# All filters and seven weight chunks loaded behind the input, the turn done by quarter products, and GpSimd's weight work moved behind the units

## The chip, the cores and the metric

The program runs on one NeuronCore of a Trainium2 chip. The metric is the device time of one execution in microseconds (us), lower being better. Matrix products run on TensorE (PE, with its weight loads as PEld), copies and elementwise work on VectorE (DVE), ScalarE (ACT) and GpSimd (POOL), and the transfers are issued mostly by SyncE (SP).

## What is computed

```python
X = np.fft.rfft(x, axis=1)                      # x: 2 x 3008 x 256
F = (filt_r + 1j * filt_i)[None, :, :]
y = np.fft.irfft(X * F, n=3008, axis=1)         # then 6016 x 256
h = y @ w_in1;  g = np.maximum(0.01 * h, h);  z = g @ w_out1    # 256 -> 2048 -> 256
h = z @ w_in2;  r = np.maximum(h, 0.0);  out = (r * r) @ w_out2
```

A filter in the frequency domain over the sequence, and two feed-forward layers behind it, all in fp32.

## The kernel before, in words

**The filter stage.** The transform of length 3008 is made of one of length 64 (N1) and one of length 47 (N2). It has these steps:

- `over_n1`: 24 groups of four fp32 products of 128x128 over the input X, written to PSUM and copied to `TT1A` (by ACT) and `TT1B` (by DVE). These arrays have two halves in their partitions (0 to 63 and 64 to 127).
- sixteen units, each of which takes eight columns of `TT1` through four steps. `turn(i)` brings the sequence index into the partitions: eight transposes against the identity, `DM[:, 2, :]`, four for each batch b, into PSUM banks 0 and 1. ACT copies the banks to S2 (`turned(i)`, line 529). `spectrum(i)` (lines 954 to 957) is four fp32 products of 48 rows and 64 columns of weights over 512 columns, one in each quarter of the array. DVE multiplies by the filter (`filtered(i)`, lines 762 and 766), POOL combines (lines 449 and 450), `inverse(i)` (lines 974 to 977) is again four quarter products, and ACT copies the result to U (`back(i)`, line 537). SP stores U to DRAM (`zu`).
- `sequence(c)` (line 997): c from 0 to 23, four fp32 products of 128x128 each, over tiles V that are loaded from `zu`. Their results are copied to YT by DVE (`Y_DVE`) and ACT (`Y_ACT`). The second half (c from 12) needs the last unit's store and a load behind it.

The order in which PE runs the units is written out by hand: in each iteration i stand `spectrum(i + 2)`, `turn(i + 3)` and `inverse(i)`, from i = 13 on with some `sequence` calls in place of the turn. ACT's order beside it is `turned(i + 3)`, then `back(i)`.

**The layers.** The products run as three fp32r passes (high and low parts of each operand) by a fast scheme with seven forms of each block of weights and tokens. For the first layer POOL makes four sums for each weight chunk k (`wi_sums`, lines 357 to 363), ACT or DVE rounds the chunk (`wi_round`), and POOL takes the low parts (`wi_split`, line 369, three instructions). The forms of the first token pair are made by DVE (lines 807 to 818) and split by `x_split0` (lines 792 and 795); each of them has to be there before a certain step of PE: `x0_lo` counts them. A slot s is one weight chunk against one pair: `up_1(s)`, `up_2(s)`, `up_6(s)`, `up_7(s)`, `up_5(s)` and `group_d(s)` (lines 1029 to 1031), with `down` (lines 1021 to 1023) some steps behind. There are 96 slots of about 10 us.

**Loads.** SP's queue runs in order. Before, it issues the input, tables and the weight chunks 0 and 1, six filters into a ring of six (`FL`), and then one filter, the unit's stores and now and then a weight chunk for each unit.

**Beside the units.** POOL makes the sums and low parts of chunks 0, 1 and the sums of chunk 2 between the units, and everything of chunks 3 to 6 right behind the last unit.

## Time and profile before

| | us |
|---|---|
| median of three runs | 1069.74 (1068.79 to 1070.24) |
| the profiled execution, device time | 1068.72 |
| its span in the trace | 1066.7 |
| PE busy in the span | 1059.6 |
| DVE, ACT, POOL busy | 755.7, 564.7, 300.7 |

TensorE had its full clock (2.4 GHz) in all forty slices of the profile. The layers take from about 101 us to the end; all that the change touches on the critical chain lies before about 107 us. A busy share says which engine has work, and the chain of waits which one sets the end: by the page, PE is 98% of it.

### The profile page before, as it was taken

What the parts mean: (1) busy time and instruction counts of PE and PEld (TensorE: products, weight loads), DVE (VectorE), ACT (ScalarE), POOL (GpSimd) and SP (SyncE); (2) the same over time, 40 slices, a digit from 0 to 9 for tenths busy, and PEclk for the clock granted to TensorE, in tenths of its full rate; (3) what the DMA queues carried; (4) which work ended last, traced back from release to release, by engine and by line L of the source; (5) the groups of instructions that cost most, each with busy time, mean ns of one, the idle gap of its engine ahead of it and who ended that gap; (6) DMA issues with size and microseconds to landing.
All of it is one profiled execution on the core that took longest, in us unless ns stands there. A gap on an engine that the chain in (4) does not pass through costs nothing.

```text
span 1066.7 us, 13987 instructions
## 1 busy us (share of the span) xinstructions
PE 1059.6 (99%) x5120; PEld 880.0 (83%) x5120; DVE 755.7 (71%) x1141; ACT 564.7 (53%) x980; POOL 300.7 (28%) x287
## 2 busy tenths in 40 slices
PE   9998999999999999999999999999999999999998
PEld 9558888888888888888999888888888888888998
DVE  2877997767767777676666767667667676676666
ACT  3666554655555555554554544544554554554443
POOL 2997552342342333332220220220220210210000
PEclk9999999999999999999999999999999999999999
DMA  9696000112112112112244000100100100100100
GB/s 321 179 298 224 10 1 1 52 36 61 47 35 68 40 42 67 38 45 57 93 160 163 21 1 1 40 1 1 40 1 1 40 1 1 40 1 1 40 1 35
DMA packets 66724, 61.45 MB, mean 58 GB/s; under 512 B 40688, under 2 KB 53856, under 8 KB 66656
## 3 DMA queue, kind: packets, MB, share of 16 engines
q1 hardware_dynamic: 66160, 60.06, 18.1%
q8 instruction: 41, 0.67, 0.3%
q10 hardware_dynamic: 496, 0.49, 0.1%
q14 instruction: 27, 0.22, 0.1%
HBM read 36.55 MB, written 23.99 MB: 57 GB/s over the span
## 4 chain that ended last, share of the span: by engine, by line
PE 98%; DVE 1%; DMA 1%; ACT 0%; issue 0%; POOL 0%; SPq 0%; DVEq 0%; ACTq 0%; POOLq 0%
PE PS L1021 16%; PE PS L1023 16%; PE PS L1022 16%; PE PS L1029 14%; PE PS L1031 14%; PE PS L1030 14%; PE PS L913 2%; PE PS L937 2%; PE PS L977 1%; PE PS L957 1%; PE PS L997 1%; DMA V<-zu 0%; PE PS L903 0%; DMA zu<-U 0%; DVE YL L792 0%; DVE XL L795 0%
## 5 line engine op out<-in xcount | busy, mean ns | idle before, releaser
L666 ACT ACTIVATE GH<-GF 128x512 fp32r<-128x512 f32 (+1 forms) x384 | 238.7, 622 | 228.0 <-DVE GF L856 116.3
L862 DVE TENSOR_TENSOR GL<-GF,GH 128x512 fp32r<-128x512 f32 (+1 forms) x384 | 260.6, 685 | 105.2 <-ACT GH L666 99.5
L1021 PE MATMUL PS<-GH,WOH 128*128 128x512 f32 (+1 forms) x768 | 296.2, 386 | 0.0
L1022 PE MATMUL PS<-GL,WOH 128*128 128x512 f32 (+1 forms) x768 | 295.8, 385 | 0.0
L1023 PE MATMUL PS<-GH,WOL 128*128 128x512 f32 (+1 forms) x768 | 295.8, 385 | 0.0
L1029 PE MATMUL PS<-XH,WIH 128*128 128x512 f32 (+1 forms) x672 | 259.8, 387 | 2.3 <-DVE XL L795 1.4
L1031 PE MATMUL PS<-XH,WIL 128*128 128x512 f32 (+1 forms) x672 | 258.8, 385 | 0.0
L830 DVE TENSOR_TENSOR GF<-PS,GF 128x512 f32<-128x512 f32 (+1 forms) x96 | 65.3, 680 | 161.7 <-ACT GF L637 161.4
L1021 PEld LDWEIGHTS PS<-GH,WOH 128*128 128x128 f32 x768 | 144.2, 188 | 28.0 <-DVE GL L862 1.5
L1023 PEld LDWEIGHTS PS<-GH,WOL 128*128 128x128 f32 x768 | 144.2, 188 | 26.9
L1022 PEld LDWEIGHTS PS<-GL,WOH 128*128 128x128 f32 x768 | 144.2, 188 | 26.8
L1029 PEld LDWEIGHTS PS<-XH,WIH 128*128 128x128 f32 x672 | 126.2, 188 | 27.1 <-DVE XL L795 1.1
L1030 PE MATMUL PS<-YL,WIH 128*128 128x512 f32 (+1 forms) x384 | 147.8, 385 | 0.0
L1031 PEld LDWEIGHTS PS<-XH,WIL 128*128 128x128 f32 x672 | 126.2, 188 | 23.6
L854 DVE SCALAR_TENSOR_TENSOR GF<-GF 128x512 f32<-128x512 f32 (+1 forms) x192 | 144.0, 789 | 1.6
L637 ACT ACTIVATE GF<-PS 128x512 f32<-128x512 f32 (+1 forms) x96 | 56.6, 589 | 163.7 <-PE PS L1023 163.7
L856 DVE SCALAR_TENSOR_TENSOR GF<-GF 128x512 f32<-128x512 f32 (+1 forms) x192 | 121.6, 674 | 1.7
L1030 PE MATMUL PS<-XL,WIH 128*128 128x512 f32 (+1 forms) x288 | 111.0, 385 | 0.0
L428 POOL TENSOR_TENSOR YL<-YT,XH 128x1024 fp32r<-128x1024 f32 (+1 forms) x22 | 52.6, 2390 | 137.8 <-DVE GL L862 137.8
L660 ACT ACTIVATE GF<-PS 128x512 f32<-128x512 f32 (+1 forms) x96 | 56.7, 591 | 57.5 <-PE PS L1031 57.5
L1030 PEld LDWEIGHTS PS<-YL,WIH 128*128 128x128 f32 x384 | 72.1, 188 | 13.3
L412 POOL TENSOR_TENSOR XT<-YT 128x512 f32<-128x512 f32 (+1 forms) x11 | 14.4, 1308 | 184.3 <-DVE GL L862 184.3
(85 smaller groups left out, 928.2 us busy)
## 6 DMA issues: line engine op xcount, KB each, us to landing
V<-zu SPq DMA_DIRECT2D x12, 512.0 KB, 6.1
zu<-U SPq DMA_DIRECT2D x31, 192.0 KB, 3.6
out_y<-YT SPq DMA_DIRECT2D x5, 1024.0 KB, 4.3
X<-in_x SPq DMA_DIRECT2D x8, 512.0 KB, 8.1
FL<-in_filt SPq DMA_DIRECT2D x16, 224.0 KB, 4.3
wi<-PWH SPq DMA_DIRECT2D x16, 224.0 KB, 2.5
wi<-PWL SPq DMA_DIRECT2D x16, 224.0 KB, 3.1
WIH<-wi SPq DMA_DIRECT2D x8, 448.0 KB, 3.5
```

Of the source, the lines that this page charges most:

```text
L660: nc.scalar.activation(GF[:, g_slot(n), 0:width(s)], PS[:, XB[s % 2], 0:width(s)], ACT.Copy).then_inc(h_sb[UD], 1)
L666: nc.scalar.activation(GH[:, g, 0:width(s)], GF[:, g, 0:width(s)], ACT.Copy).then_inc(g_hi[kind], 1)
L830: nc.vector.tensor_tensor(h, PS[:, YB, 0:w], h, ALU.add).then_inc(h_sb[UA], 1)
L854: nc.vector.scalar_tensor_tensor(h, h, 0.01, h, ALU.mult, ALU.max).then_inc(g_sb[kind], 1)
L856: nc.vector.scalar_tensor_tensor(h, h, 0.0, h, ALU.max, ALU.mult).then_inc(g_sb[kind], 1)
L862: nc.vector.tensor_tensor(GL[:, g, 0:w], GF[:, g, 0:w], GH[:, g, 0:w].bitcast(f32), ALU.subtract).then_inc(g_lo[kind], 1)
L1021: nc.tensor.matmul(acc, wh, xh, start=first, stop=False)
L1022: nc.tensor.matmul(acc, wh, xl, start=False, stop=False)
L1023: return nc.tensor.matmul(acc, wl, xh, start=False, stop=last)
L1029: nc.tensor.matmul(acc, wh, xh, start=first, stop=False, skip_group_check=not first)
L1030: nc.tensor.matmul(acc, wh, lo, start=False, stop=False, skip_group_check=not first)
L1031: return nc.tensor.matmul(acc, wl, xh, start=False, stop=True, skip_group_check=not first)
```

## The change

It has five parts.

- **Turn by quarter products.** Each of the eight transposes of 128x112 becomes four products of 64 rows, 48 columns of weights and 64 columns of identity, one in each quarter of the array: `h` is the half of the partitions, `part` the parity. The result of half h goes to bank h, so that a bank now holds both batches. ACT's two copies each read one bank as before in size, but both wait for the end of the whole turn (four counts), where before the first waited for the first four transposes. The two MEMSETs of the padding go, and the eight warm-up products write two banks.
- **Loads.** The filters have a place each: ten in the later home of the weight forms, six in the place of the ring. All sixteen are issued behind the input, with the weight chunks 1 to 6 among them, and the units' part of the queue holds only stores and V.
- **POOL beside the units.** Only the sums of chunk 1 remain there, behind units 13 and 14. Behind the last unit come the sums of 2 and 3, the split of 1, sums of 4, split of 2, sums of 5, then a wait for four of the first pair's splits (`x0_lo`), the splits of 3 and 4, and the rest in later slots behind `after_splits`.
- **The last two units.** The U copy of unit 14 is shared by ACT and DVE, as that of unit 15 was before.
- **First pair.** DVE makes the fifth split before `whole_a(0)`; ACT rounds the chunks 3, 4 and 5 there, and 6 and 7 in slots 2 and 4.

The diff, cut to its core:

```diff
@@ SP
-            load_w1i(1)
-            for i in range(FSLOTS):
+            for i in range(UNITS):
                 load_filter(i)
-                if i == 2:
-                    load_w1i(2)
+                if i >= 3 and i - 2 < WI_SEAM:
+                    load_w1i(i - 2)
             for i in range(UNITS):
-                if i + FSLOTS < UNITS:
-                    load_filter(i + FSLOTS)
                 store_u(i)
-                if i in (1, 2, 4, 6):
-                    load_w1i(WI_EARLY + (1, 2, 4, 6).index(i))
@@ POOL
-            def beside_psum(s):
-                pool.wait_ge(g_lo[UB], s)
+            def after_splits(s):
+                pool.wait_ge(g_lo[UC], s - 1)
@@ ACT
             def turned(i):
-                for b in range(B):
-                    act.wait_ge(s2_ps, 2 * i + b + 1)
-                    nc.scalar.activation(S2[:, i % 2, b, :, :].rearrange("p j d -> p (j d)"), PS[0:KR, b, :], ACT.Copy).then_inc(s2_sb, 1)
+                act.wait_ge(s2_ps, 4 * i + 4)
+                for h in range(2):
+                    nc.scalar.activation(S2[:, i % 2, :, :, 64 * h:64 * h + 64].rearrange("p b j d -> p (b j) d"),
+                                         PS[0:KR, h, :].rearrange("p (n d) -> p n d", d=64), ACT.Copy).then_inc(s2_sb, 1)
...
             def wi_round(k):
                 act.wait_ge(wi_s, 4 * k + 4)
+                act.wait_ge(wi_hi, k)
@@ DVE
-            wi_round(WI_EARLY - 1)
+            wi_round(1)
+            back(UNITS - 2)
             dve.wait_ge(yf_sb, 2 * UNITS)
             y_copy(1)
...
+            back(UNITS - 1)
+            wi_round(2)
             y_copy(5)
@@ PE, turn(i)
+                if i >= 1:
+                    pe.wait_ge(s2_sb, 2 * i)
                 for b in range(B):
-                    if i >= 1:
-                        pe.wait_ge(s2_sb, 2 * i - 1 + b)
                     for k in range(UJ):
                         q = 2 * (UJ * u + k)
-                        mm = nc.tensor.transpose(PS[0:KR, b, 128 * k:128 * k + 128],
-                                                 TT1[half][:, b, q:q + 2, :].rearrange("p q r -> p (q r)")[:, 0:KR], DM[:, 2, :])
-                    mm.then_inc(s2_ps, 1)
+                        for h in range(2):
+                            d = slice(64 * h, 64 * h + 64)
+                            c = 64 * (UJ * b + k)
+                            for part in range(2):
+                                mm = nc.tensor.matmul(PS[IM * part:IM * part + R, h, c:c + 64], TT1[half][d, b, q + part, 0:R],
+                                                      DM[d, 2, d], start=True, stop=True)
+                                if b == B - 1 and k == UJ - 1:
+                                    mm.then_inc(s2_ps, 1)
```

TensorE's order in one iteration of the units (spectrum, turn, inverse), before:

```order
L957 MATMUL PS<-S_60,TW 64x512 [waits prod,s2_sb]
L957 MATMUL PS<-S_60,TW 64x512 x3
L937 MATMUL PS<-DM,TT1A 112x128 [waits s2_sb]
L937 MATMUL PS<-DM,TT1A 112x128 x3
L937 MATMUL PS<-DM,TT1A 112x128 [waits s2_sb]
L937 MATMUL PS<-DM,TT1A 112x128 x3
L977 MATMUL PS<-AF_52,TW 64x512 [waits u_sb,yf_sb]
L977 MATMUL PS<-AF_52,TW 64x512 x3
```

and after (line 956 is the new turn):

```order
L977 MATMUL PS<-S_61,TW 64x512 [waits prod,s2_sb]
L977 MATMUL PS<-S_61,TW 64x512 x3
L956 MATMUL PS<-DM,TT1A 48x64 [waits s2_sb]
L956 MATMUL PS<-DM,TT1A 48x64 x31
L1000 MATMUL PS<-AF_52,TW 64x512 [waits u_sb,yf_sb]
L1000 MATMUL PS<-AF_52,TW 64x512 x3
```

The sequence of steps is the same; eight instructions with two waits have become thirty-two with one. ScalarE beside it, before (two copies of the turn, each with a wait of its own, and two of U):

```order
L529 ACTIVATE S_60<-PS 112x512 [waits s2_ps] x2
L537 ACTIVATE U<-PS 112x512 [waits u_ps]
L537 ACTIVATE U<-PS 112x512
L529 ACTIVATE S_60<-PS 112x512 [waits s2_ps] x2
L537 ACTIVATE U<-PS 112x512 [waits u_ps]
```

and after:

```order
L540 ACTIVATE S_61<-PS 112x8x64 [waits s2_ps]
L540 ACTIVATE S_61<-PS 112x8x64
L549 ACTIVATE U<-PS 112x512 [waits u_ps]
L549 ACTIVATE U<-PS 112x512
L540 ACTIVATE S_61<-PS 112x8x64 [waits s2_ps]
L540 ACTIVATE S_61<-PS 112x8x64
```

Only the first copy of a turn has a wait left, and that is one for the whole turn. GpSimd behind the last unit (the last pair of lines 449 and 450), before:

```order
L450 TENSOR_TENSOR AF_50<-AF_50,BF_53 112x512
L369 TENSOR_TENSOR WIL<-WIF,WIH 128x384 [waits wi_hi]
L369 TENSOR_TENSOR WIL<-WIF,WIH 128x256 [waits wi_hi] x2
L357 TENSOR_TENSOR WIF<-WIF 128x128 [waits wi_raw3]
L359 TENSOR_TENSOR WIF<-WIF 128x128 [waits wi_s]
L362 TENSOR_TENSOR WIF<-WIF 128x128 [waits wi_s]
L363 TENSOR_TENSOR WIF<-WIF 128x128
```

and after, from the sums of chunk 3 to the wait for the first pair's splits:

```order
L355 TENSOR_TENSOR WIF<-WIF 128x128
L361 TENSOR_TENSOR WIL<-WIF,WIH 128x384 [waits wi_hi]
L361 TENSOR_TENSOR WIL<-WIF,WIH 128x256 [waits wi_hi] x2
L349 TENSOR_TENSOR WIF<-WIF 128x128 [waits wi_raw4]
...
L361 TENSOR_TENSOR WIL<-WIF,WIH 128x256 [waits wi_hi] x2
L349 TENSOR_TENSOR WIF<-WIF 128x128 [waits wi_raw5]
L351 TENSOR_TENSOR WIF<-WIF 128x128 [waits wi_s]
L354 TENSOR_TENSOR WIF<-WIF 128x128 [waits wi_s]
L355 TENSOR_TENSOR WIF<-WIF 128x128
L361 TENSOR_TENSOR WIL<-WIF,WIH 128x384 [waits wi_hi,x0_lo]
```

Before, one split and then four chunks' sums follow the last unit; after, four chunks' sums (2 to 5) with two splits among them, then the new wait.

## Rows read from the trace of the kernel before

**Rows 1.** The table by stretch: window, length, each engine's busy us (instructions), clock, DMA.

```profile
80.00:100.00 20.00, 17.74 (x140) 16.34 (x138) 14.58 (x18) 13.67 (x23) 18.20 (x25) 1.00 0.83 299
...
120.00:140.00 20.00, 20.00 (x89) 16.30 (x88) 18.41 (x23) 12.24 (x20) 10.71 (x7) 1.00 0.00 1
```

**Rows 2.** The timeline of one unit: start, length, engine, line, tiles [idle before, releaser].

```profile
43.20 1.04 PE L957 MATMUL PS<-S,TW 48*64 48x512 f32 x8
...
44.17 1.09 PE L937 MATMUL PS<-DM,TT1A 128*112 128x128 f32 x8
...
44.86 1.09 ACT L529 ACTIVATE S<-PS 112x512 f32<-112x512 f32 x2 [0.24 <-PE PS L937]
...
45.19 1.09 PE L977 MATMUL PS<-AF,TW 48*64 48x512 f32 x8
...
45.99 0.26 PEld L957 LDWEIGHTS PS<-S,TW 48*64 48x64 f32 x8 [0.60 <-ACT S L529]
46.10 1.04 PE L957 MATMUL PS<-S,TW 48*64 48x512 f32 x8
```

**Rows 3.** The timeline at the first turn and spectrum, TensorE alone.

```profile
23.81 1.06 PE L937 MATMUL PS<-DM,TT1A 128*112 128x128 f32 x8
...
25.70 0.43 PE L954 MATMUL PS<-S,TW 48*64 48x256 f32 x1
...
25.75 0.13 PEld L954 LDWEIGHTS PS<-S,TW 48*64 48x64 f32 x1
...
25.96 0.40 PE L954 MATMUL PS<-S,TW 48*64 48x256 f32 x2
```

**Rows 4.** Groups by line and shape up to 110 us: busy, mean ns of one.

```profile
L957 PE MATMUL PS<-S,TW 48*64 48x512 f32 x120 | 16.8, 594 | 0.0
```

**Rows 5.** The timeline at the last unit, number 15.

```profile
69.31 1.04 PE L957 MATMUL PS<-S,TW 48*64 48x512 f32 x8
...
71.70 1.40 DVE L766 SCALAR_TENSOR_TENSOR BF<-PS,SG,FL 112x512 f32<-112x512 f32 x2
...
73.18 1.57 POOL L449 TENSOR_TENSOR AF<-AF,BF 112x512 f32<-112x512 f32 x1 [0.39 <-DVE BF L766]
...
74.71 1.27 POOL L450 TENSOR_TENSOR AF<-AF,BF 112x512 f32<-112x512 f32 x1
...
76.83 1.09 PE L977 MATMUL PS<-AF,TW 48*64 48x512 f32 x8 [0.28 <-ACT U L537]
```

**Rows 6.** The timeline of GpSimd behind the last unit.

```profile
75.94 2.36 POOL L369 TENSOR_TENSOR WIL<-WIF,WIH 128x384 fp32r<-128x384 f32 x3
...
78.27 0.45 POOL L357 TENSOR_TENSOR WIF<-WIF 128x128 f32<-128x128 f32 x1
...
80.15 0.46 POOL L357 TENSOR_TENSOR WIF<-WIF 128x128 f32<-128x128 f32 x1
```

**Rows 7.** The timeline between the units and the layers: ScalarE, VectorE and TensorE.

```profile
80.55 0.68 DVE L807 TENSOR_TENSOR XT<-YT 128x512 f32<-128x512 f32 x1
...
86.65 0.95 ACT L547 ACTIVATE WIH<-WIF 128x896 fp32r<-128x896 f32 x1 [0.91 <-POOL WIF L363]
...
90.02 1.14 DVE L813 TENSOR_TENSOR XT<-YT,XT 128x512 f32<-128x512 f32 x1 [0.83 <-ACT YT L543]
...
92.32 1.37 DVE L792 TENSOR_TENSOR YL<-YT,XH 128x512 fp32r<-128x512 f32 x1
...
93.75 0.50 PE L1029 MATMUL PS<-XH,WIH 128*128 128x512 f32 x1 [0.82 <-DVE YL L792]
```

**Rows 8.** The timeline at the layers' first slot: GpSimd's splits, TensorE and VectorE.

```profile
86.58 12.10 POOL L369 TENSOR_TENSOR WIL<-WIF,WIH 128x384 fp32r<-128x384 f32 x12
...
100.43 0.50 PE L1029 MATMUL PS<-XH,WIH 128*128 128x512 f32 x1 [0.92 <-DVE XL L795]
...
103.20 0.68 DVE L838 TENSOR_TENSOR GF<-PS,GF 128x512 f32<-128x512 f32 x1
...
104.33 0.47 PE L1029 MATMUL PS<-XH,WIH 128*128 128x512 f32 x1
```

More of the change, by code:

```diff
@@ L104, in fft_mlp_kernel @@
         warm_sb = sem("warm_sb")
-        ft_in = [sem(f"ft_in{g}") for g in range(FSLOTS)]
+        ft_in = [sem(f"ft_in{i}") for i in range(UNITS)]
         tw_in = sem("tw_in")
@@ L441, in _ @@
                 wi_split(0, part)
-            for part in range(2):
-                wi_sums(1, part)
             for i in range(UNITS):
@@ L535, in back @@
                     act.wait_ge(z_out[i % RINGS], 32 * (i // RINGS))
-                for js in range(2 if i < UNITS - 1 else 1):
+                for js in range(2 if i < UNITS - 2 else 1):
                     nc.scalar.activation(U[:, i % RINGS, 2 * js:2 * js + 2, :].rearrange("p j e -> p (j e)"), PS[0:KR, 6 + js, :], ACT.Copy).then_inc(u_sb, 1)
@@ L901, in _ @@
             pe.wait_ge(warm_sb, 1)
-            for _ in range(8):
-                nc.tensor.matmul(PS[:, 0, 0:128], WARM[:, :], WARM[:, :], start=True, stop=True)
+            for h in range(2):
+                for k in range(UJ):
+                    nc.tensor.matmul(PS[:, h, 128 * k:128 * k + 128], WARM[:, :], WARM[:, :], start=True, stop=True)
             pe.wait_ge(dft_in, 16)
```

129 lines of the change are left out of this document (74 added, 55 removed).

## The prediction

> **What bounds the kernel now.** I read the page first: TensorE is busy for 1059.6 of 1066.7 us and makes 98% of the chain, so a change can give back little except where TensorE waits or does avoidable work. The layers, from about 101 us on, are one unbroken run of TensorE; nothing that the change touches shortens them. What remains is the first 101 us. There the table by stretch shows TensorE at 17.74 of 20 us between 80 and 100 [rows 1], and the timeline shows what it does in a unit.
>
> One unit takes from 43.20 to 46.10, 2.90 us [rows 2]. The spectrum starts at 43.20, the turn at 44.17, the inverse at 45.19, the next spectrum at 46.10: steps of 0.97, 1.02 and 0.91. A step of four quarter products is two passes over 512 columns. With the record at a mean of 594 ns [rows 4], and 0.91 from inverse to spectrum of which about 0.05 is the first weight load, a pass streams for 0.43, and 0.165 is the way out of the array. The spectrum's 0.97 is therefore 0.86 and a gap of 0.11 before the turn, and the turn's 1.02 holds another 0.15 or so of first load and emptying.
>
> The second thing to see in rows 2 is how little room ScalarE leaves. Its two copies of the turn take 1.09 together (44.86 to 45.95), and the next spectrum's weights are loaded at 45.99, "0.60 <-ACT S". The products then start at 46.10, when the inverse has left the array. So ScalarE's chain is only about 0.05 shorter than TensorE's, and it is that short only because its first copy starts 0.69 after the turn does, in the middle of it.
>
> **Turn by quarter products.** A product of 64 columns streams for an eighth of 0.43, 0.054. Each quarter has eight products of two passes, so sixteen rounds, 0.056 each with a little for the start: 0.89 in all, against 0.87 of pure streaming of the eight transposes. What goes is the change of layout on both sides, 0.11 and 0.15. TensorE's own time for a unit would be 0.86 + 0.89 + 0.86 = 2.61 in place of 2.90. Over sixteen units that alone would be 4.6 us gained.
>
> But the chain through ScalarE gets longer. Let the turn start at 0. Its last round starts at 0.84 and leaves the array after 0.054 + 0.165, with 0.02 for the fourth quarter: 1.08. ScalarE starts 0.03 later (the first four transposes ended 0.03 before 44.86 by the same reckoning), 1.11. Both copies have the size that they had, 1.09: 2.20. The load of the spectrum's weights follows 0.04 later, and its first products 0.05 behind that: 2.29. The spectrum takes 0.86 and the next turn stands behind it in TensorE's order. The period is 3.15, and the inverse (0.86) fits into the hole, in which TensorE idles for about 0.5. ScalarE has no backlog: copies of U begin at 2.2 and end at 3.3, and the next turn is ready for it at 4.3. VectorE, which keeps up with 2.90 and has waits in it, and GpSimd (two operations at 1.3, [rows 5]) fit into 3.15 too.
>
> So a unit costs 0.25 **more**, not 0.29 less. From the first spectrum (25.70 before) to the sixteenth (69.31 before, [rows 5]) there are fifteen periods, and the first turn to its spectrum takes 2.29 in place of 1.9 (23.81 to 25.70, [rows 3]): the last spectrum starts at 25.7 + 0.37 + 15 x 3.145 = 73.25. **Term 1: +3.95 us** (bounds 3.4 and 4.6, from 0.03 either way on ScalarE's start and the weight loads).
>
> The Trainium skill has two rules that bear on these small products. Its page "TensorEngine Tiling (Array Packing)", Key Properties, says that a change of tiling mode drains the engine; the 0.11 and 0.15 of rows 2 agree, and by that rule alone the change would be worth the 4.6 us above. The page "TensorE: Matmul & The Clock Gate", Part 3, says that weight loads overlap running products only where the row group differs. The rows speak against it: at 25.75 a second load of the same kind is under way while the first product (25.70, 0.43 long) still runs in each quarter, and the second passes follow at 25.96 without a hole [rows 3].
>
> **Loads.** Sixteen filters and six chunks, by their shapes 3.6 and 1.5 MB, come behind the input of 6.2 MB. At the 300 GB/s that the queue moves when it is full [rows 1], they land by about 38 us, one filter each 1.5 us at most, where a unit asks for one each 3.15 us and the first at 27 us. Nobody waits for them before or after. Later the queue has only stores and V, which wait for nobody either except the last store and the loads behind it, and those follow an empty queue in both kernels. I take 0, with -0.5 as the bound.
>
> **The last unit.** Call D the moment when VectorE has done unit 15: 73.10, 3.79 behind its spectrum [rows 5]. Before, GpSimd ends at D + 2.88 and the inverse starts at 76.83, D + 3.73, after a wait for the copy of U. That wait goes, since VectorE takes one of the two copies. In its place come the sums of chunk 1: four instructions at 1.9 for all (78.27 to 80.15, [rows 6]). The first two hold up unit 14 by some 0.5, the other two end at D + 0.8, and unit 15 on GpSimd at D + 3.6. The inverse starts at D + 3.7. Term 2: 0.
>
> **Between units and layers.** Before, VectorE makes and splits the first pair's forms while GpSimd splits weights (86.58 for 12.10, [rows 8]). An operation that takes 0.68 alone (80.55) takes 1.14 and 1.37 beside GpSimd [rows 7], and TensorE waits for them, 0.82 before 93.75 [rows 7] and 0.92 before 100.43 [rows 8]. The change holds GpSimd back at that point. From 90.02 to the split at 93.69 there are three operations and a small wait; at 0.70 each it would be 2.1 in place of 3.7 (92.32 + 1.37 - 90.02), a gain of 1.6, and over all of the forms up to 100.43 some 2.8.
>
> What is late next is ScalarE. The rounding of the last early chunk waited 0.91 for GpSimd's sums at 86.65, and the y copies that the forms need are queued behind it, the last of them done at 90.0 [rows 7]. Before, the sums of chunk 6 were done at D + 13.5. Now ScalarE waits for the sums of chunk 5, and before them stand, from D + 3.6: four chunks' sums at 1.9 and two splits at 2.4, 12.4 us and some 0.6 for meeting VectorE. That is D + 16.6. The y copy that starts the forms is done at D + 20.0 instead of D + 16.9: 3.1 later. The wait that was taken from VectorE comes back as a wait for GpSimd. Followed on: the split that TensorE needs for `up_2(0)` comes at D + 22.2 (before D + 20.6), and `up_5(0)` at D + 27.2 (before 100.43, D + 27.3), because the forms then run at their free pace. Behind that GpSimd's splits of chunks 3 and 4, about 6 us beside VectorE, fall on the sixth and seventh forms and the first split of g. `whole_b(0)`, at 103.20 before (D + 30.1, done 30.8), ends at D + 32.2, and `group_d(0)`, at 104.33 (D + 31.2), starts then; TensorE's own work would let it start at D + 30.9. **Term 3: +0.5**, bounds -0.3 (TensorE's own work) and +1.1 (VectorE's chain), and I take the middle, nearer to the upper end, because the meeting of GpSimd and VectorE is seen in each row of that place.
>
> **In the layers** GpSimd has the splits of chunks 5 and 6 and the sums of 6 more, 6.7 us in slots 2 to 6. VectorE has room there in the trace, and TensorE does not wait. I take 0; bounds -0 and +4.
>
> **The sum.** 1068.7 (the profiled execution) + 3.95 + 0 + 0.5 = 1073.2. The median of the three runs stands 1.0 above the profiled execution, so a median after it would be **1074.2 us**.
>
> **The rivals.**
>
> *The gap between units and layers is won in full* (not slower). TensorE lacks 2.3 of 20 us from 80 to 100 [rows 1] and 0.4 behind it, 2.7 in all, and up to 3.4 with the holes that the records' tails hide. If GpSimd's sums of chunk 5 come before ScalarE asks (the point is D + 13.5) or if the copies behind are not what the forms wait for, this comes back, and 3.95 - 3.4 = +0.5 is left: 1070.3. Against it: 12.4 us of GpSimd's work cannot end by D + 13.5 when it begins at D + 3.6. Chance 0.15.
>
> *The thirty-two products take longer.* If a quarter's weight load (48 columns; one of 64 shows about 0.05) did not run under the products, a round would take 0.10 and a turn 1.55, and the period would be 3.8: 10 us more, 1084. By the skill's Part 3 rule named above this is what would happen. For it: sixteen short rounds in a row are nowhere in this trace. Against it: rows 3, and starts of products and loads within 0.09 us for all quarters. Chance 0.12.
>
> *VectorE falls behind in the first pass.* It is busy for 18.41 of 20 us from 120 to 140 [rows 1], and the 6.7 us come on top; should each us cost it 0.5, it is at its limit and TensorE loses 2 to 4 us beside the sum: 1077. Chance 0.06.
>
> *ScalarE's copies do not bind*, the period is TensorE's 2.61, and the gain of 4.6 stands: 1065 to 1066. It needs the copies to overlap the turn, which the wait for all four counts forbids. Chance 0.05, with everything else that could make it faster.
>
> *The forecast*: 0.62, on its own 1071.7 to 1076.5.
>
> A measurement of this kernel can tell about 0.2%, 2.1 us, from no change. Slower by more than that: the forecast but for a small part, the long turn and the late VectorE, 0.77. Within it: the first rival and the rest of the forecast, 0.17. Faster: 0.06. The range reaches from 1069.8 to 1081.
>
> **What would show it.** Right: in the timeline the spectra are 3.1 to 3.2 apart; ScalarE's copy of the turn starts 1.1 behind the turn; TensorE's weight loads of the spectrum wait for "ACT S", now with TensorE idle for 0.5; the turn itself takes about 0.9 and is followed by the inverse without a gap; ScalarE waits some 2 to 3 us for GpSimd's sums before its last early rounding; the forms take 0.7 each. Wrong: a period below 2.9 (the copies overlap after all), a turn above 1.1, a `group_d(0)` less than 27 us behind the last unit's D, or waits of TensorE in slots 2 to 6.

## The result

The changed kernel takes 1082.33 us (median of 4 runs, 1081.65 to 1083.18) against 1069.45 for the kernel before. The ratio is 1.0121, with a 95% interval from 1.0109 to 1.0134. The forecast was 1074.2 and its range ended at 1081.0, so the direction was right and the size was not: +12.9 us in place of +4.5.

The profile after has a span of 1079.5 us, 12.8 more than before. Below are lines of its page: busy time by engine, the granted clock and DMA share in 40 slices, and the queues (packets, MB, share).

```profile
PE 1061.9 (98%) x6016; PEld 884.5 (82%) x6016; DVE 833.0 (77%) x1142; ACT 561.6 (52%) x979; POOL 316.9 (29%) x285
...
PE   9888999999999999999999999999999999999998
...
DMA  9768100112112212212244100100100000100100
...
q8 instruction: 48, 0.79, 0.3%
```

TensorE's 896 additional records cost it hardly any busy time (1061.9 against 1059.6). What is new is idle time, in the second and third slices, 27 to 81 us, which stand at 8 where the page of before has 9 (the fourth has 8 in both). The last line has an odd item: queue 8 carries instructions, in blocks of 16 KB, and there are 48 where the page of before has 41:

```profile
q8 instruction: 41, 0.67, 0.3%
```

**The steady unit.** This is the timeline of TensorE and ScalarE over one unit, with columns as in rows 2.

```profile
51.78 1.09 PE L977 MATMUL PS<-S,TW 48*64 48x512 f32 x8 [0.42 <-ACT S L540]
...
52.69 1.07 PE L956 MATMUL PS<-DM,TT1A 64*48 64x64 f32 x64
...
53.59 1.04 PE L1000 MATMUL PS<-AF,TW 48*64 48x512 f32 x8
53.91 1.08 ACT L540 ACTIVATE S<-PS 112x512 f32<-112x512 f32 x2 [1.21 <-PE PS L956]
...
55.05 0.21 PEld L977 LDWEIGHTS PS<-S,TW 48*64 48x64 f32 x8 [1.30 <-ACT S L540]
55.05 1.09 PE L977 MATMUL PS<-S,TW 48*64 48x512 f32 x8 [0.42 <-ACT S L540]
```

The period is 55.05 - 51.78 = 3.27, where rows 2 had 2.90 and the forecast 3.15. The turn takes 0.90 to the inverse, as forecast. ScalarE's copies start 1.22 behind the turn's start (forecast 1.11), and the next spectrum starts 1.14 behind them.

**The first units.** Here TensorE stops, first in the middle of a spectrum and then in the middle of a turn.

```profile
29.98 1.08 PE L977 MATMUL PS<-S,TW 48*64 48x512 f32 x5 [0.18 <-ACT S L540]
32.41 0.64 PE L977 MATMUL PS<-S,TW 48*64 48x512 f32 x2 [1.36 <-issue]
...
34.90 2.07 PE L929 MATMUL PS<-DM,X 128*128 128x128 f32 x8
...
37.85 0.84 PE L956 MATMUL PS<-DM,TT1A 64*48 64x64 f32 x44
40.24 0.48 PE L956 MATMUL PS<-DM,TT1A 64*48 64x64 f32 x18 [1.55 <-issue]
```

Neither stop has a releaser ("issue": the engine waited for nothing that the profile shows), and between the two the `over_n1` group takes 2.07 us. The table by stretch says why that group is slow (last columns: granted clock, DMA share, GB/s):

```profile
32.00:34.00 2.00, 1.59 (x49) 1.20 (x53) 0.41 (x1) 0.00 (x0) 1.13 (x1) 0.90 1.06 269
34.00:36.00 2.00, 2.00 (x34) 1.85 (x27) 2.00 (x3) 1.00 (x2) 0.00 (x0) 0.50 1.08 271
36.00:38.00 2.00, 2.00 (x25) 1.19 (x28) 0.13 (x1) 0.69 (x2) 1.79 (x2) 0.74 1.07 267
38.00:40.00 2.00, 0.69 (x48) 0.54 (x37) 1.75 (x2) 0.00 (x0) 0.71 (x1) 1.00 1.03 266
```

After the first stop the clock falls to 0.50 (1.2 GHz) for about 3.4 us (33.6 to 37.0), while the load queue is full. Rows 1 to 8 have nothing like it.

**Behind the units.** The timeline of what waits:

```profile
97.42 0.95 ACT L560 ACTIVATE WIH<-WIF 128x896 fp32r<-128x896 f32 x1 [2.63 <-POOL WIF L355]
101.64 0.95 ACT L560 ACTIVATE WIH<-WIF 128x896 fp32r<-128x896 f32 x1 [2.84 <-POOL WIF L355]
103.22 2.92 PE L1020 MATMUL PS<-DM,V 128*128 128x128 f32 x24 [1.22 <-ACT YT L555]
104.75 0.69 DVE L827 TENSOR_TENSOR XT<-YT,XT 128x512 f32<-128x512 f32 x1 [3.80 <-ACT YT L555]
...
106.94 0.50 PE L1052 MATMUL PS<-XH,WIH 128*128 128x512 f32 x1 [0.80 <-DVE YL L801]
...
120.31 0.50 PE L1052 MATMUL PS<-XH,WIH 128*128 128x512 f32 x1 [1.19 <-DVE GF L862]
```

The form that took 1.14 at 90.02 [rows 7] takes 0.69 (L827), since GpSimd rests, and it starts later, since ScalarE's y copies stand behind roundings that wait for GpSimd. D, the moment when VectorE has done unit 15, is 85.02. The second rounding starts at D + 16.6, as forecast. `up_2(0)` is at D + 21.9 (forecast 22.2), `up_5(0)`, at 111.74, at D + 26.7 (forecast 27.2), and `group_d(0)`, at 116.82, at D + 31.8 (forecast 32.2). The wait of 1.19 at 120.31 is one that the forecast did not have.

**Where the 12.8 us are.** The last spectrum starts at 81.19 instead of 69.31 [rows 5], 11.9 later. Of these, 0.5 lie ahead of the first turn, in `over_n1` (the clock rose to full at 6.30 instead of 5.36 us; over all the kernels here it rose between 3.9 and 6.9), 0.5 lie between the first turn and its spectrum (24.31 to 26.71, against 23.81 to 25.70 in rows 3), and 15 x (3.267 - 2.907) = 5.4 are the period. The rest, 5.5, are the two stops with the half clock behind them. What follows the units adds about 1.0: TensorE is 14.0 behind the kernel before at 120 us, and 1.1 of it comes back by 372 us.

### The profile page after: what moved, and what is told of

Its sections match the earlier page's. It is cut to its first block, busy times and chain, and to the rows that moved or that the text cites. A ratio compares the mean times of both kernels' runs of the same rounds, so it can differ in the third digit from the quotient of the medians.

```text
span 1079.5 us, 15784 instructions
## 1 busy us (share of the span) xinstructions
PE 1061.9 (98%) x6016; PEld 884.5 (82%) x6016; DVE 833.0 (77%) x1142; ACT 561.6 (52%) x979; POOL 316.9 (29%) x285
## 4 chain that ended last, share of the span: by engine, by line
PE 93%; POOL 2%; DVE 2%; ACT 1%; issue 1%; DVEq 0%; POOLq 0%; ACTq 0%
PE PS L1045 16%; PE PS L1044 16%; PE PS L1046 16%; PE PS L1052 14%; PE PS L1053 14%; PE PS L1054 14%; PE PS L929 2%; PE PS L956 2%; PE PS L977 1%; ACT S L540 1%; POOL WIL L361 1%; DVE GF L869 0%; POOL AF L440 0%; PE PS L919 0%; POOL AF L439 0%
## 5 line engine op out<-in xcount | busy, mean ns | idle before, releaser
L877 DVE TENSOR_TENSOR GL<-GF,GH 128x512 fp32r<-128x512 f32 (+1 forms) x384 | 272.1, 711 | 109.9 <-ACT GH L677 103.0
L869 DVE SCALAR_TENSOR_TENSOR GF<-GF 128x512 f32<-128x512 f32 (+1 forms) x192 | 171.2, 932 | 1.6
L871 DVE SCALAR_TENSOR_TENSOR GF<-GF 128x512 f32<-128x512 f32 (+1 forms) x192 | 159.2, 870 | 1.7
```

The costliest lines, as they stand in the source:

```text
L869: nc.vector.scalar_tensor_tensor(h, h, 0.01, h, ALU.mult, ALU.max).then_inc(g_sb[kind], 1)
L871: nc.vector.scalar_tensor_tensor(h, h, 0.0, h, ALU.max, ALU.mult).then_inc(g_sb[kind], 1)
L877: nc.vector.tensor_tensor(GL[:, g, 0:w], GF[:, g, 0:w], GH[:, g, 0:w].bitcast(f32), ALU.subtract).then_inc(g_lo[kind], 1)
```

## Experiments

Unless said otherwise a kernel is the changed one with the edit shown, and all times are medians. Theory F, formed from the two stops: TensorE's instructions come over the DMA engines that also carry the data, the quarter products use them up fast, and under a full load queue the next block comes late. Theory C: the period is the chain from turn to copy to spectrum. Theory T: behind the units GpSimd holds ScalarE, and so the y copies.

### x1_spread: the loads as before

```diff
-            for i in range(UNITS):
-                load_filter(i)
-                if i >= 3 and i - 2 < WI_SEAM:
-                    load_w1i(i - 2)
+            load_w1i(1)
+            for i in range(6):
+                load_filter(i)
+                if i == 2:
+                    load_w1i(2)
             for i in range(UNITS):
+                if i + 6 < UNITS:
+                    load_filter(i + 6)
                 store_u(i)
+                if i in (1, 2, 4, 6):
+                    load_w1i(3 + (1, 2, 4, 6).index(i))
```

> The changed kernel, but with the loads where they were before: six filters and the weight chunks 1 and 2 behind the input, the other ten filters and four chunks one by one in the units. The places in SBUF stay those of the changed kernel. After has 5.5 us in which TensorE stands or runs at half clock between 30 and 42 us, while the DMA share is 1.0. Theory F (TensorE's instructions are fetched by the same DMA engines; thirty-two short products a turn use them up, and under the full load queue the next block comes too late): both holes and the half clock are gone, the first five spectra are 3.27 apart, and the time is 1082.3 - 5.5 = 1076.8. Rival R1 (the number of instructions alone makes the holes, whatever the loads do): the holes stay, 1082. Rival R2 (the loads alone slow TensorE): as F here; the run with transposes tells them apart.

Measured: 1076.67 (1076.09 to 1078.04), ratio 1.0063 [1.0048, 1.0078]. Of the stops one is left, a small one (0.8 us from one start to the next), at the same products of the same spectrum; then all periods are 3.26 to 3.28. The number of instructions alone, rival R1, does not make the long stops.

```profile
30.50 0.13 PEld L982 LDWEIGHTS PS<-S,TW 48*64 48x64 f32 x2 [1.09 <-issue]
```

### x2_transp: the transposing turn under the early loads

```diff
-                                mm = nc.tensor.matmul(PS[IM * part:IM * part + R, h, c:c + 64], TT1[half][d, b, q + part, 0:R],
-                                                      DM[d, 2, d], start=True, stop=True)
+                        mm = nc.tensor.transpose(PS[0:KR, b, 128 * k:128 * k + 128],
+                                                 TT1[half][:, b, q:q + 2, :].rearrange("p q r -> p (q r)")[:, 0:KR], DM[:, 2, :])
```

The copies, the counts, the warm-up products and the memsets of the padding are those of before too.

> The changed kernel with the turn of before: eight transposes, a copy for each batch with its own wait, the padding. All loads stay behind the input. F: with 8 instead of 32 products in a turn no block of instructions is late, the period is 2.90 again, and what is left of the change is the tail, +1.0: 1070.5. R2 (the loads alone slow TensorE): holes between 30 and 42 us here too, 1074 or more. If the first rival of the prediction held in part (tail won), below 1069.

Measured: 1070.76 (1070.20 to 1071.94), ratio 1.0012 [1.0002, 1.0022]. There is no stop, although the queue is as full (DMA share 1.06 from 28 to 40 us), and the periods are 2.89 to 2.96, so the loads alone, rival R2, are out too.

### x6_transp_spread: the weight work alone

Both edits above together.

> The kernel before with the change's weight work alone: the turn by transposing products and the loads spread as before, and of the change only what GpSimd, VectorE and ScalarE do with the weights between and behind the units. Against before it shows the tail's part of the change, against the change with the transposing turn and early loads (1070.8 us) the early loads' part. Theory F (early loads cost only where small products use up instructions fast): the same as with early loads, 1070.3 to 1071.3 us. Rival L (early loads have a price or a gain of their own): off by over 1 us from 1070.8.

Measured: 1070.84 (1069.99 to 1071.27), ratio 1.0014 [1.0004, 1.0023]. This fills a square of four kernels that all have the change's weight work:

| | loads spread | loads early |
|---|---|---|
| transposing turn | 1070.84 | 1070.76 |
| quarter products | 1076.67 | 1082.33 |

The early loads cost nothing with the transposing turn and 5.7 us with the quarter products. The weight work by itself costs 1.3 (1070.84 against 1069.5 of before in the shared runs).

### x3_onecount: one count for a turn

```diff
-                                if b == B - 1 and k == UJ - 1:
+                                if b == B - 1 and k == UJ - 1 and h == 1 and part == 1:
                                     mm.then_inc(s2_ps, 1)
...
-                act.wait_ge(s2_ps, 4 * i + 4)
+                act.wait_ge(s2_ps, i + 1)
```

> The changed kernel with one count for a turn, on its very last product, in place of four on the last product of each quarter. In after ScalarE starts 1.22 behind the turn, 0.15 behind the end of the last product's record; before it was 0.03. If the four counts one behind the other cost this, ScalarE starts at 1.12 to 1.15, the period falls from 3.27 to about 3.18, and over sixteen units 1.3 to 1.6 us come back: 1080.9. If the late start belongs to the quarter products themselves, the period stays 3.27 and the time 1082.3. The holes between 30 and 42 us stay in both.

Measured: 1081.69 (1080.88 to 1083.62), ratio 1.0111 [1.0096, 1.0126]. The period is 3.19, and ScalarE's copy starts 1.15 behind the turn. The other three counts are worth 0.08 of a period. In the time of the whole that is not to be told from none (-0.6, the ranges overlap). The profiled execution is the slowest of the four; in it the second stop takes 3.3 us from one start to the next, against 1.8 in the changed kernel, and half clock for 6.8 us follows.

### x5_turnonly: the kernel before with the quarter-product turn

The reverse of the turn's edit, made to the kernel before: loads and weight work stay.

> The kernel before with the quarter-product turn alone: all loads, GpSimd's order, rounding and the last units as before. ScalarE's chain theory: period 3.27 from the first unit, the last spectrum 5.4 + 0.5 later than before, nothing else: 1069.4 + 5.9 = 1075.3, no hole by F since the loads are spread. R1: holes as in after, 1081. If ScalarE's chain were not what sets the period in after but the shifted work of GpSimd or the loads: period 2.9 or less, 1065 to 1069.

Measured: 1075.17 (1074.64 to 1075.62), ratio 1.0047 [1.0032, 1.0062]. The period is 3.27 again. Against the 1069.7 of before in the same runs, the turn by itself costs 5.5 of the 12.9 us. There is no stop: the block that lands at 28.98 is there just in time for the place where the changed kernel stops first, which TensorE passes at 30.50 here.

### x4_spread_reorder: TensorE's turn ahead of the spectrum

```diff
                 if i + 3 < UNITS:
                     turn(i + 3)
+                if i + 2 < UNITS:
+                    spectrum(i + 2)
```

The spectrum's call ahead of it goes, and the loads are spread.

> The change with the loads spread as before (1076.7 us), and in TensorE's program each turn(i+3) stands ahead of spectrum(i+2) in the loop of units instead of behind it. No instruction is added or taken away. Theory C (the unit's period is set by ScalarE's copies: turn, copy of PS to S, spectrum stand in one chain with nothing of TensorE's between turn and copy): with the spectrum of the unit before between a turn and its own spectrum, TensorE no longer waits for the copy, the wait behind ACT's S goes from 1.2 to 1.3 us to under 0.3, and the period from 3.27 to what the rest allows, 2.6 to 2.9 us; 14 periods make 5 to 9 us: 1068 to 1072 us. Rival P (the quarter products themselves, or their issue, set the period): it stays at 3.2 to 3.3 us, 1076.7 us. If the gain comes, instructions of TensorE are also used up faster, and by theory F (late instruction fetch) a hole of 1 to 3 us may stand in the units.

Measured: 1075.10 (1074.76 to 1075.82), ratio 1.0054 [1.0039, 1.0069]. A unit in its timeline:

```profile
60.85 1.09 PE L961 MATMUL PS<-DM,TT1B 64*48 64x64 f32 x64
...
61.74 1.05 PE L982 MATMUL PS<-S,TW 48*64 48x512 f32 x8
62.16 1.09 ACT L545 ACTIVATE S<-PS 112x512 f32<-112x512 f32 x2
62.60 1.55 PE L1005 MATMUL PS<-AF,TW 48*64 48x512 f32 x7
```

Turn to spectrum 0.89, spectrum to inverse 0.86: TensorE no longer waits for the copy. Six of the fifteen periods are 2.62 to 2.64, close to the 2.61 that the prediction gave as TensorE's own work. Theory C holds, and rival P does not. The others are 2.15 (the last), 2.8 to 3.65 and once 5.11, with a stop in the second spectrum (0.82 without a weight load). In some of the longer ones the inverse waits for GpSimd's AF (seven waits with 4.5 us in all from 36 to 74 us). Two hold further short stops without a releaser:

```profile
44.14 0.31 PE L961 MATMUL PS<-DM,TT1A 64*48 64x64 f32 x2 [0.33 <-issue]
...
49.58 0.71 PE L961 MATMUL PS<-DM,TT1B 64*48 64x64 f32 x35 [0.35 <-issue]
```

The last spectrum starts at 72.53, 3.6 sooner than in x1_spread, but the time is only 1.6 less: GpSimd ends unit 15 at 81.25 and in x1_spread at 83.09, and the y copies wait for its sums behind that. Half of the gain in the units is lost to GpSimd's queue.

### x9_burst and x9b_burst_transp: a full queue in the middle of the units

```diff
+                if i == 3:
+                    act.dma_start(scr, x[:, 0:1, :, :]).then_inc(scr_done, 16)
                 back(i)
```

> The change with the loads spread as before (1076.7 us), and one extra copy of 3.1 MB from memory to memory, which nothing uses, put into the DMA queues by ScalarE in unit 3, so that the queues are full in the middle of the units, where the change has them full at the start. Theory F (TensorE's instructions come over the same DMA engines as the data, and the many small products use them up sooner than a block comes under a full load): a hole of 1 to 3 us with nothing to wait for stands in TensorE's row in the middle units, half clock behind it, 1 to 5 us longer: 1078 to 1082. Rival S (holes belong to the first units, the start of the program, or to the filters' own arrival, not to load on the queues): no hole, 1076.7 to 1077.

> As the last kernel (transposing turn, loads spread), with the extra copy of 3.1 MB put into the DMA queues in unit 3, as in the run with the quarter products, where a hole of over 2 us stood at 57 us and half clock behind it. Theory F (a late instruction block needs both a full queue and many small products): no hole, at most 1 us over the same kernel without the copy. Rival D (the copy disturbs the units in another way, by transfers that the units themselves need, such as filters): a wait of some engine for a transfer, 2 us or more over it.

Measured: 1082.15 (1081.76 to 1084.81), +5.5 over x1_spread; and 1079.07 (1077.61 to 1080.43), +8.2 over x6_transp_spread. The second contradicts what theory F expected of it, and rival D was right: the copy delays the units' own transfers.

```profile
55.24 1.08 ACT L558 ACTIVATE U<-PS 112x512 f32<-112x512 f32 x2 [5.77 <-DMA zu<-U]
```

So the two times cannot be compared as I had meant. The traces still differ in kind. With the transposing turn the one long stop of TensorE (4.73 before 56.47) waits for this copy, and half clock comes with it too (0.50 from 54.5 to 61.3). With the quarter products the first stop is one in the middle of a turn, with 62 of its 64 records done and nothing to wait for, so rival S, by which no such stop would come in the middle units, is out. Only then come waits for a filter and a store, which are part of the 5.5:

```profile
58.91 0.31 PE L966 MATMUL PS<-DM,TT1B 64*48 64x64 f32 x2 [2.32 <-issue]
...
62.18 1.23 DVE L783 TENSOR_TENSOR AF<-PS,FLA 112x1024 f32<-112x1024 f32 x1 [3.73 <-DMA FLA<-in_filt]
63.26 1.08 ACT L556 ACTIVATE U<-PS 112x512 f32<-112x512 f32 x2 [2.92 <-DMA zu<-U]
...
60.00:64.00 4.00, 3.30 (x76) 2.08 (x72) 1.82 (x3) 1.08 (x3) 1.02 (x1) 0.62 1.07 385
```

### x14_waits_early and x14b_waits_spread: padding

```diff
+                        for _ in range(14):
+                            pe.wait_ge(warm_sb, 1)
                         mm = nc.tensor.transpose(PS[0:KR, b, 128 * k:128 * k + 128],
```

> The change with the transposing turn (1070.8 us, early loads, no hole), and ahead of each of the eight products of a turn fourteen waits on a semaphore that was reached long before: 112 more instructions in a unit, as many as the quarter products add with their weight loads, and no other work. Theory F (holes come where TensorE's instructions are used up faster than they arrive under the full load queue): a hole of 1 us or more with nothing to wait for stands in TensorE's row in the first five units, though no quarter product is there, and half clock may follow; 2 to 8 us longer than the same padding with spread loads. Rival Q (the holes belong to the quarter products themselves): no hole, the same as with spread loads. The padding by itself may take 10 to 30 ns an instruction, 1 to 3 us a unit where it is not hidden; the comparison is with the next kernel.

> The same padding of 112 satisfied waits in a unit with the loads spread as before. Theory F: no hole, or at most a small one in units 1 and 2 as with the quarter products and spread loads; 2 to 8 us less than with early loads. Rival Q: the same as with early loads, within 1 us.

Measured: 1144.43 and 1144.42, two executions each. The times decide nothing: the padding had a price of its own that I had put too low.

```profile
125.17 0.43 PE L956 MATMUL PS<-DM,TT1B 128*112 128x128 f32 x1 [0.33 <-issue]
125.97 0.43 PE L956 MATMUL PS<-DM,TT1B 128*112 128x128 f32 x1 [0.37 <-issue]
```

Products of a turn stand about 0.8 apart, at half clock as here and at full clock (24.05 to 29.63) alike. In the trace fourteen waits are seven instructions of up to two waits each, 0.106 us apart, so a wait that is already satisfied takes some 53 ns. A unit thus has 56 instructions more and not the 112 that I wanted. The units take 7.4 us, most of it at half clock, and the instruction blocks come 13 to 20 us apart, so the padding used instructions up more slowly than the quarter products do. The experiment failed to make the condition that it was for.

### What settles theory F: when the blocks land

The trace records each 16 KB packet of queue 8. Taken together over the kernels they show a thing that no single kernel did. Each row is one stop of TensorE with no releaser; from one start to the next these stops are 0.5 to 3.3 us long. The last column is the place in the program: how many of TensorE's records (products, weight loads and waits, as the trace has them) stand ahead of the one with which it goes on.

| kernel | block's packet, us | TensorE goes on at | behind its end | records ahead |
|---|---|---|---|---|
| after | 29.61 to 30.94 | 32.41 | 1.47 | 705 |
| after | 37.68 to 38.92 | 40.24 | 1.32 | 961 |
| x3_onecount | 29.68 to 31.03 | 32.57 | 1.54 | 705 |
| x3_onecount | 37.91 to 39.10 | 40.56 | 1.46 | 961 |
| x1_spread | 27.87 to 29.00 | 30.50 | 1.50 | 705 |
| x4_spread_reorder | 28.77 to 29.85 | 31.27 | 1.42 | 705 |
| x4_spread_reorder | 41.86 to 42.82 | 44.13 | 1.32 | 1473 |
| x4_spread_reorder | 47.22 to 48.28 | 49.58 | 1.30 | 1729 |
| x9_burst | 29.27 to 30.37 | 31.83 | 1.46 | 705 |
| x9_burst | 56.23 to 57.38 | 58.91 | 1.53 | 1985 |

All ten stops end 1.3 to 1.5 us behind a block. Five of them are at the same place in the program, ahead of the last three products of the second spectrum, whatever the time, and the other five stand exactly 256, 768, 1024 or 1280 records further on, whole multiples of 256. So a block holds 256 of TensorE's instructions, and it stops at the edge of one, when the next has not come. The counts of the whole program agree: 10473 records of TensorE and 41 blocks before, 12265 and 48 after, a difference of 1792 records, 7 times 256. The queue's line in the window 29.5 to 31.0 of the changed kernel is this, and in the window 31.0 to 37.5 the instruction queue has no line at all:

```profile
q8 instruction: 1, 0.02, 5.5%
```

With quarter products and spread loads a block comes each 4 to 6 us (27.87, 31.61, 36.25, 42.09 in x1_spread). In the changed kernel the one behind 29.61 comes at 37.68, 8 us later, and TensorE runs dry. With the transposing turn a block comes each 12 to 16 us (30.87, 42.98, 58.55 in x2_transp), and lateness of a few us has no effect. The windows 27 to 66 us of x1_spread and 26 to 66 us of the kernel before show the same rates:

```profile
q8 instruction: 8, 0.13, 1.2%
```

```profile
q8 instruction: 3, 0.05, 0.5%
```

How late a block comes can be read too. When TensorE passes an edge (449, 705, 961 records and so on), the next packet of queue 8 follows, and the time between the two depends on how full the DMA engines are:

| kernel | edge passed at | next packet after | DMA share between |
|---|---|---|---|
| after | 24.76 | 4.8 | 1.07 |
| after | 32.41 | 5.3 | 1.07 |
| x1_spread | 30.50 | 1.1 | 0.00 |
| x1_spread | 35.16 | 1.1 | 0.00 |
| x9_burst | 36.49 | 0.9 | 0.00 |
| x9_burst | 52.47 | 3.8 | 1.01 |
| x2_transp | 27.40 | 3.5 | 1.07 |
| x14_waits_early | 29.31 | 4.9 | 1.07 |
| x14b_waits_spread | 28.78 | 1.2 | 0.15 |

In all eight kernels with early loads and in none of the others the packet behind the edge at 24 to 30 us comes under a share of 1.07, and it takes 3.5 to 5.0 us there, and 5.3 at the next edge in the two that stop. (In x1_spread the one behind 24.01 takes 3.9 as well, since the input is still arriving.) Where the share is a third or less, up to 50 us, it takes 1.3 at most. So the blocks are late under the transposing turn and under the padding as well (x2_transp, x14_waits_early); there 256 instructions last 14 us and more, and nobody notices. The padded pair thus bears theory F out after all, though not by its times. The trace has no row for the request itself; that it is made about when an edge is passed is inferred from these times.

### x7_round5: one rounding moved out of ScalarE's way

On x2_transp:

```diff
-                if c in (6, 8, 10):
+                if c in (6, 8):
                     wi_round(WI_EARLY + (c - 6) // 2)
...
+                if s == 1:
+                    wi_round(WI_SEAM - 2)
```

> The change with the transposing turn (1070.8 us), and ScalarE's sixth rounding of inner weights moved out of slot 0 into slot 1, behind the y copies. Theory T (behind the units TensorE in slots 0 and 1 waits for y copies that stand in ScalarE's queue behind roundings which wait 2.6 and 2.8 us for GpSimd's sums): the y copies of slot 0 start up to 2.8 us sooner, and TensorE's waits behind ScalarE there (1.2 us at the last one) go: 1 to 2 us faster, 1069 to 1069.8 us. Rival: VectorE's forms, not ScalarE's copies, set these slots, and the time stays at 1070.8.

Measured: 1067.74 (1067.11 to 1071.11), ratio to before 0.9985 [0.9976, 0.9995]; 3.0 less than x2_transp. In x2_transp the y copies stood behind this:

```profile
90.61 0.95 ACT L562 ACTIVATE WIH<-WIF 128x896 fp32r<-128x896 f32 x1 [2.84 <-POOL WIF L358]
91.47 0.58 ACT L557 ACTIVATE YT<-PS 128x512 f32<-128x512 f32 x1
```

Now they start where TensorE ends, and the wait of VectorE for them falls from 4.27 to 0.83:

```profile
91.02 0.69 DVE L831 TENSOR_TENSOR XT<-YT,XT 128x512 f32<-128x512 f32 x1 [0.83 <-ACT YT L557]
```

Theory T holds, and it was worth more than the 1 to 2 us expected. It stands below the kernel before by 0.15%, and so, by 0.1%, do x10_round5_late and x12_best, which have the same rounding in slot 1; none of the three can be told from the others.

### x8_late and x10_round5_late: GpSimd kept off VectorE

```diff
-            pool.wait_ge(x0_lo, 4)
-            for k in (3, 4):
-                for part in range(3):
-                    wi_split(k, part)
+            pool.wait_ge(x0_lo, 7)
             wo_split(0)
             wo_split(1)
+            for k in (3, 4):
+                for part in range(3):
+                    wi_split(k, part)
```

The first on x2_transp, the second on x7_round5.

> The change with the transposing turn (1070.8 us), and GpSimd's splits of inner chunks 3 and 4 stand behind its first two outer splits, all held until VectorE has done its seven forms of x, so that GpSimd rests while VectorE works on the first slots. Theory G (GpSimd's work beside VectorE's stretches the latter's forms from 0.7 to 1.1 to 1.8 us, and TensorE's waits of 1.0 and 1.2 us at the first group and down products are behind these): those two waits shrink, 1 to 2 us faster, 1069 to 1069.8. Rival: the delayed splits come late for ScalarE or TensorE and a new wait takes the place, 1071 or more. Second rival: the waits were covered by others, 1070.8.

> The change with the transposing turn, the sixth inner rounding in slot 1 (1067.7 us), and GpSimd's splits of inner chunks 3 and 4 behind its first outer splits, all held until VectorE has done its seven forms of x. By itself the last step gave nothing (1071.1 against 1070.8), since the y copies then set slot 0. With those out of the way, theory G expects VectorE's forms of 0.7 instead of over 1 us to count: 0.5 to 1.5 us faster, 1066.2 to 1067.2. Rival: the first group and down products wait for the inner chunks' splits, 1068 or more.

Measured: 1071.12 and 1068.13, against 1070.76 and 1067.74 without the edit. No gain, even where the y copies are out of the way. In x7_round5 the waits are 0.62 at the first group product and 1.16 some 3.5 us behind it. With the splits shifted, another wait takes their place, as the rival said, though VectorE's split of g releases it (first x8_late, then x10_round5_late):

```profile
114.28 0.50 PE L1041 MATMUL PS<-GH,WOH 128*128 128x512 f32 x1 [1.75 <-DVE GL L879]
```

```profile
111.55 0.50 PE L1043 MATMUL PS<-GH,WOH 128*128 128x512 f32 x1 [1.74 <-DVE GL L881]
```

### x15_round45: the rounding before it as well

```diff
-                if c in (6, 8):
-                    wi_round(WI_EARLY + (c - 6) // 2)
+                if c == 6:
+                    wi_round(WI_EARLY)
...
                 if s == 1:
+                    wi_round(WI_SEAM - 3)
                     wi_round(WI_SEAM - 2)
```

> The version at 1067.7 us (transposing turn, the change's weight work and early loads, sixth inner rounding in slot 1), and the fifth rounding moved to slot 1 as well. ScalarE waited 2.8 us for GpSimd's sums ahead of it at 86.9 us, but the y copy behind it stood only 0.8 us ahead of VectorE's wait. Theory T: 0.3 to 0.8 us faster, 1067.0 to 1067.4. Rival: the splits of that chunk, which GpSimd makes behind the rounding, come late for the first down product of its step: 1068.5 or more.

Measured: 1076.56 (1075.66 to 1077.68), 8.8 more than x7_round5. The rival was right, and through a queue that I had not named:

```profile
113.76 0.79 PE L1044 MATMUL PS<-GH,WOH 128*128 128x512 f32 x1 [7.72 <-POOL WOL L369]
...
110.00:115.00 5.00, 1.24 (x3) 1.05 (x4) 0.00 (x0) 1.00 (x2) 4.87 (x6) 0.50 0.00 0
```

GpSimd's in-order queue has the splits of chunk 4 ahead of the first outer splits. They wait for the rounding, the outer splits wait behind them, and TensorE's first product of the second layer waits for those. TensorE then works at half clock until about 120 us, which is part of the 8.8.

### x12_best: both orders together

The transposing turn, spread loads, x7's rounding and x4's order.

> Transposing turn, loads spread as before, the change's weight work, ScalarE's sixth inner rounding in slot 1 (1067.7 us with early loads), and TensorE's turn(i+3) ahead of spectrum(i+2). Theory C: with the transposing turn the copies' chain bounds the period of 2.90 us too, so the order by itself takes it to about 2.62, as it did with the quarter products where no instruction came late; 14 periods give 4 us in the units, of which GpSimd's sums behind the units may keep 1 to 2: 1063.5 to 1066 us. By theory F no hole stands in the units. Rival: with the transposing turn TensorE's own work, with its modes drained between products, is the bound and the period stays 2.9: 1067.7.

Measured: 1068.23 (1067.90 to 1068.94), the same as x7_round5. The rival holds here: the period stays 2.89, and now TensorE itself is the bound.

```profile
43.05 1.08 PE L961 MATMUL PS<-DM,TT1A 128*112 128x128 f32 x8
...
44.06 1.09 PE L981 MATMUL PS<-S,TW 48*64 48x512 f32 x8
...
44.97 1.04 PE L1004 MATMUL PS<-AF,TW 48*64 48x512 f32 x8
```

The steps are 1.01, 0.91 and 0.97 (the next turn is at 45.94), 2.89 in all, with no wait for a copy. A unit of 2.62 in x4_spread_reorder has 0.90, 0.86 and 0.86 (its turn is at 37.10, then 37.99, 38.86 and 39.71). So the quarter products do save 0.27 of TensorE's own time in a unit. Of this, 0.22 lie in the two steps with a change of layout, into the turn and out of it, and 0.05 between spectrum and inverse, where nothing changes; no run takes the change of layout alone. The order by itself gives the transposing turn nothing.

## Why the prediction was right and wrong

**Term 1, the period: mechanism right, size short.** The forecast said that ScalarE's copies, now behind a whole turn, set the period. That is what the waits show, x4_spread_reorder shows it by taking the chain apart, and x5_turnonly by itself has it in another kernel. The step was +0.25 a unit and measured +0.36. ScalarE started 1.22 behind the turn, not 1.11, 0.08 of it by the four counts in place of one (x3_onecount), which I had not costed at all. Fifteen periods and the first turn measured 5.9 where the term had 3.95, outside its bounds of 3.4 and 4.6. (The sum's 0.37 for the first turn should have been 2.29 - 1.89 = 0.40; it measured 0.51.)

**The 2.61 of TensorE's own work: right**, seen as 2.62 to 2.64 once the chain no longer bound it. The rule of the Trainium skill's page "TensorEngine Tiling (Array Packing)", Key Properties, that a change of tiling mode drains the engine, agrees with the 0.22 that the two steps with a change of layout take longer in x12_best. The rule of the Trainium skill's page "TensorE: Matmul & The Clock Gate", Part 3, that weight loads overlap running products only where the row group differs, does not agree: the 64 records of a turn start within 0.90, where the prediction had 1.55 for loads that do not hide.

**"Loads": the step that failed.** I wrote that nobody waits for the loads and took 0, with -0.5 as the bound. No instruction waits for a filter, and that much is right. But I asked only who waits for the transfers themselves, and not what else travels on the same engines. TensorE's instructions do: they come in blocks of 256, the queue that is full until 40 us holds each block back by 3.5 to 5.3 us, and TensorE stops at the edge. The page of before had the row (41 blocks of the instruction queue), and with 1792 more records of TensorE the rate in the units more than doubles. The term of 0 measured 5.5 in the profiled execution, 5.7 by x1_spread. That is 5.5 of about 8.4 us missed on the profiled execution's terms; the period is 1.9, the tail 0.5 and the later start of its first turn 0.5. The landing time was a little off as well: the full queue moved 268 GB/s and not 300, and emptied at about 40.5 us instead of 38.

**Half clock** was in no part of the sum. It follows from the stops: the rows show it behind a stop of TensorE, from 33.6 to 37.0 us in the changed kernel and from 61.0 to 71.2 in x9_burst. It costs at most half of the 3.4 us in the changed kernel, 1.7 of the 5.5 (an estimate).

**Term 2: right.** The last inverse started at D + 3.4 (forecast 3.7).

**Term 3: the mechanism right, at its upper bound.** +1.0 in the profile, 1.3 by x6_transp_spread, where I had 0.5 with bounds -0.3 and +1.1. The gain on VectorE's forms came (0.69 each) and ScalarE's waits for GpSimd took it back (2.6 and 2.8 us), as written. x7_round5 confirms the wait: with the second rounding out of the way 3.0 us come back, about its 2.84. At `group_d(0)`, the point that the sum took, the loss was 0.6, as forecast; a wait at 120.31 that the forecast did not have added 1.5, and 1.1 of the whole came back later. That the end shows 1.0 is in part luck.

**In the layers: right.** VectorE was 77 us busier (833.0 against 755.7), and TensorE lost nothing by it: the shift against the kernel before goes from 14.0 at 120 us to 12.9 at 372 us and stays there to the end.

**Of the rivals** none came true. "The thirty-two products take longer" had a time near the measured one (1084) by a wrong mechanism; the turn itself took 0.90.

## What to carry to other kernels

When a change multiplies the number of small instructions on one engine, count the instructions that it needs in the dense stretch (here 256 to a block of the instruction queue in the table of DMA queues), and ask what else fills the DMA engines then; a load that no instruction waits for can still stop an engine. Before replacing an engine's work by faster work, ask whether the copy behind it can start in the middle of it, and if not, put other work of the engine between them. Work taken off one engine's queue should not leave an instruction in another in-order queue that waits ahead of what is urgent: moving one rounding gave 3.0 us, moving the next cost 8.8.

## What was not expected of the hardware

- TensorE stops without a releaser and goes on 1.3 to 1.5 us behind the end of a 16 KB packet of the instruction queue, in ten stops of five kernels, all at whole multiples of 256 of its instructions from each other.
- Such a packet comes 3.5 to 5.3 us behind the passing of a block's edge where the early loads fill the DMA engines, and 1.3 us at most where they are mostly idle.
- Fourteen waits on a semaphore that had long been reached put 0.8 us between two products, some 53 ns a wait, and they are not hidden.
- Four products that each raise a semaphore, in place of one, cost ScalarE's start 0.07 to 0.08 us.
- A stop of 1.4 us with little work around it was followed by some 3.4 us at 1.2 GHz.
